# A new beginning for a fused linear-attention and two-layer kernel: fewer warm-up matmuls, moved state sums, loads behind the masks, and decay scans run backwards

## The reference, cut to what matters

```python
for t in range(S):                                   # attention, S = 768
    cur = einsum('bhd,bhe->bhde', u[None] * kt, vt)
    y[:, :, t] = einsum('bhd,bhde->bhe', rt, state + cur)
    state = wt[:, :, :, None] * state + einsum('bhd,bhe->bhde', kt, vt)
...
h = x @ w_in                                         # 384 -> 2048
g = h * clip(h + 3.0, 0.0, 6.0) / 6.0
x = g @ w_out                                        # 2048 -> 384
...
xn = x / sqrt(mean(x * x) + 1e-06) * rms_g
g = xn @ w_gate; val = xn @ w_val                    # 384 -> 1536, twice
out = (silu(g) * val) @ w_out2                       # 1536 -> 384
```

## Time and profile before

| | |
|---|---|
| median of 3 runs | 933.13 us (932.55 to 935.83) |
| the profiled execution | 935.66 us, of which 933.9 us are its span |
| PE busy | 921.6 us, 99% of the span |
| DVE, ScalarE (ACT), POOL busy | 521.3, 361.7, 291.9 us |
| moved by DMA | 60.40 MB |
| mean granted TensorE clock | 0.998 |

### The profile page before, as it was taken

How to read it: one execution, slowest core, us unless ns; L and a number is a source line. 1 busy time by engine, 2 the same in 40 slices (tenths; PEclk the granted TensorE clock), 3 DMA queues, 4 the chain that set the end, 5 groups by cost and what they waited for, 6 DMA issues and landing times.

```text
span 933.9 us, 17547 instructions
## 1 busy us (share of the span) xinstructions
PE 921.6 (99%) x7064; PEld 772.9 (83%) x7064; DVE 521.3 (56%) x752; ACT 361.7 (39%) x786; POOL 291.9 (31%) x244
## 2 busy tenths in 40 slices
PE   7999999999999999999999999999999999999998
PEld 7899988888888888888888888888888888888886
DVE  6888976566666666315774553553463373363332
ACT  4557454354444445336463123223223223223212
POOL 4789544454454444324351011011011001101000
PEclk9999999999999999999999999999999999999999
DMA  9874442233223231014221010010000001000000
GB/s 255 237 208 129 109 131 60 63 105 86 75 61 107 69 83 51 22 39 135 86 83 45 0 35 34 1 34 34 0 34 35 1 19 50 0 1 34 1 1 34
DMA packets 33008, 60.40 MB, mean 65 GB/s; under 512 B 6112, under 2 KB 19936, under 8 KB 32928
## 3 DMA queue, kind: packets, MB, share of 16 engines
q1 hardware_dynamic: 27104, 50.82, 18.7%
q10 hardware_dynamic: 5824, 8.47, 3.1%
HBM read 47.66 MB, written 9.44 MB: 61 GB/s over the span
## 4 chain that ended last, share of the span: by engine, by line
PE 93%; DVE 4%; issue 1%; DMA 1%; ACT 1%; SPq 1%; DVEq 0%; ACTq 0%
PE acc L1079 34%; PE bank L1050 11%; PE bank L1052 11%; PE bank L1051 11%; PE pair L1050 5%; PE pair L1051 5%; PE pair L1052 5%; DVE ki L731 1%; PE acc L1113 1%; PE pair L1132 1%; PE pair L1189 1%; PE pair L1161 1%; DVE cum L719 1%; PE bank L1068 1%; PE bank L1153 1%
## 5 line engine op out<-in xcount | busy, mean ns | idle before, releaser
L1079 PE MATMUL acc<-gs,w_dn 128*128 128x512 f32 (+1 forms) x1512 | 357.0, 382 | 1.2 <-issue 1.2
L1079 PEld LDWEIGHTS acc<-gs,w_dn 128*128 128x128 f32 x1512 | 272.9, 188 | 55.1 <-issue 1.3
L945 POOL TENSOR_TENSOR gs<-act_g,gs 128x512 fp32r<-128x512 f32 (+1 forms) x96 | 122.1, 1272 | 208.3 <-ACT gs L550 208.2
L1050 PE MATMUL bank<-xs,w_up 128*128 128x512 f32 (+1 forms) x459 | 171.9, 374 | 1.4 <-DVE state L762 1.2
L1052 PE MATMUL bank<-xs,w_up 128*128 128x512 f32 (+1 forms) x459 | 169.1, 368 | 0.0
L1051 PE MATMUL bank<-xs,w_up 128*128 128x512 f32 (+1 forms) x459 | 169.0, 368 | 0.0
L801 DVE SCALAR_TENSOR_TENSOR act_g<-act_u,bank 128x512 f32<-128x512 f32 (+1 forms) x112 | 67.5, 603 | 139.8 <-ACT act_u L542 139.8
L869 DVE TENSOR_TENSOR act_u<-act_u,bank 128x512 f32<-128x512 f32 x72 | 49.5, 688 | 146.8 <-ACT act_u L612 146.8
L542 ACT ACTIVATE act_u<-bank,half 128x512 f32<-128x512 f32 (+1 forms) x112 | 70.0, 625 | 150.8 <-PE bank L1052 139.9
L616 ACT ACTIVATE gs<-act_g 128x512 fp32r<-128x512 f32 x72 | 45.5, 632 | 155.9 <-DVE act_g L875 155.9
L1050 PEld LDWEIGHTS bank<-xs,w_up 128*128 128x128 f32 x459 | 86.4, 188 | 18.0 <-DVE state L762 1.6
(11 more groups left out here) (121 smaller groups left out, 1121.6 us busy)
## 6 DMA issues: line engine op xcount, KB each, us to landing
rkn<-in_rkN SPq DMA_DIRECT2D x22, 384.0 KB, 4.1
rkt<-in_rkT SPq DMA_DIRECT2D x44, 192.0 KB, 3.6
val<-in_valN SPq DMA_DIRECT2D x22, 256.0 KB, 3.0
x<-x_dram SPq DMA_DIRECT2D x6, 768.0 KB, 4.2
dec<-in_decT SPq DMA_DIRECT2D x46, 97.5 KB, 2.3
x_dram<-xo SPq DMA_DIRECT2D x5, 768.0 KB, 4.1
out<-xo SPq DMA_DIRECT2D x5, 768.0 KB, 3.3
raw_dn<-in_w_out SPq DMA_DIRECT2D x14, 192.0 KB, 4.8
```

Of the source, the lines that this page charges most:

```text
L945: pool.tensor_tensor(gs[:, f % GRING, 1, tok], act_g[:, f % 2, tok], gs[:, f % GRING, 0, tok].bitcast(F32), ALU.subtract).then_inc(s_glo, 1)
L1050: pe.matmul(dst, w_hi, x_hi, start=first, stop=False)
L1079: last = pe.matmul(ps_o[m][:, tok], w[:, wp, m * P:(m + 1) * P], gs[:, f % GRING, xp, tok], start=f == 0 and a == 0, stop=f == nf - 1 and ...
```

## The change

The decays of a chunk are no longer inverted. `prep_suffix` runs one scan backwards over the raw decays, and its result, the product of all decays behind a step, multiplies the keys directly. Its value at the chunk's start is the product over the whole chunk. `prep_prefix` takes the reciprocal of that one value (112 x 8 elements) and runs a second scan, forwards and in place over `dec`, that starts from it. POOL multiplies the queries by that. Per group, four reciprocals of 112 x 128 leave, and one scan of 112 x 520 and one reciprocal of 112 x 8 come. Because `dec` is overwritten, all groups load 64 rows of its first half (48 before), and its next load waits for `s_rd` instead of `s_cum` and stands one group later. `update_state` adds for every group, and `scale_state` runs for groups 0 and 1 too.

At the beginning PE issues 10 matmuls on ones (3 of 512 columns, 7 of 128) instead of 30 of 128. `sums(0)` and the DVE work behind it move into slice 0 of pass 0, and `keys(1)` into slice 2. The copies of values (`place_val3`), the first copy of keys and half of the second bonus fill move from ScalarE to DVE. ScalarE issues the loads of up slices 0 to 2 and of `u_b`. SP waits for both masks (`s_mask` 2) before it issues the loads of group 2, of up slice 3, and all behind them.

```diff
 # SyncE, before pass 0
-            landed(sp, ldR, 1, 2)
-            for b in range(PB):
-                sp.dma_start(u_b[...], ...)
-            load_rkn(2)
-            load_dec(2)
+            load_dec(2)
+            sp.wait_ge(s_mask, 2)
+            load_rkn(2)
+            load_up(sp, EARLY_UP)          # EARLY_UP = 3
+            load_dn(sp, 0)
             load_rk(2)
-            sp.wait_ge(s_ki, 2)
-            for f in range(FIRST_UP, FIRST_UP + 2):
+            load_dn(sp, 1)
+            for f in range(EARLY_UP + 1, FIRST_UP + 2):
                 load_up(sp, f)
                 load_dn(sp, f - 2)
             load_dec(3); load_rkn(3); load_rk(3)
 # VectorE
+            def prep_suffix(g):
+                dve.tensor_tensor_scan(suffix[...][:, ::-1], dec[::-1], first1[::-1], 1.0, ALU.mult, ALU.add)
+            def prep_prefix(g):
+                dve.reciprocal(whole1[0:DP, :, :, 0:1], whole(g))
+                dve.wait_ge(s_inv, g + 1)
+                dve.tensor_tensor_scan(dec, dec, whole1, 1.0, ALU.mult, ALU.add)
...
             for g in range(2):
-                prep_scan(g)
-                for part in range(2):
-                    prep_inv(g, part)
+                prep_suffix(g)
+                prep_prefix(g)
                 prep_k(g)
             dve.wait_ge(const, NCONST)
             for g in range(2):
-                mask_scores(g)
+                place_val3(g)
+            copy_first_keys()
+            mask_scores(0)
+            fill_half()
+            mask_scores(1)
...
                 if phase == INV1 and g + 3 < GROUPS:
-                    prep_scan(g + 3)
-                if phase in (INV1, INV2) and g + 3 < GROUPS:
-                    prep_inv(g + 3, phase - INV1)
+                    prep_suffix(g + 3)
+                if phase == INV2 and g + 3 < GROUPS:
+                    prep_prefix(g + 3)
 # GpSimd
-            pool.wait_ge(s_cum, 2)
             rk_mul(1)
 # TensorE
-            busy(20)
+            busy(3, 4)
+            busy(5, 1)
             bonuses(0)
-            busy(3)
             scores(0)
             keys(0)
-            busy(3)
+            busy(2, 1)
             bonuses(1)
-            sums(0)
-            busy(4)
             scores(1)
             outputs(0)
             outputs(1)
-            keys(1)
...
+                    if (e, f) == (0, 0):
+                        pe.wait_ge(s_bonus, PLACED)
+                        sums(0)
                     if (e, f) == (0, 2):
-                        sums_read(pe, 0)
+                        keys(1)
```

More of the change, by code:

```diff
@@ L99, in build @@
         first1 = sa("first1", [P, PAIRS, PB, T1])
[L100 removed]
+        whole1 = sa("whole1", [P, PAIRS, PB, T1])
+        suffix = sa("suffix", [P, 2, CHUNKS + 2])
         rd = sa("rd", [P, 2, PAIRS, PB, T])
@@ L160, in key_bank @@
         def key_bank(g):
-            return ps_h[g] if g < 2 else ps_c
+            return ps_h[0] if g == 0 else ps_c
         def sum_bank(g, b):
@@ L212, in columns, with after, whole @@
             return slice(g % B * C, (g % B + 1) * C)
-        def is_first(g):
-            return g < SETS
+        def after(g):
+            return suffix[0:DP, slot(g), 2:2 + CHUNKS].rearrange("p (c t) -> p c t", t=T1)[:, :, 0:T]
+        def whole(g):
+            return suffix[0:DP, slot(g), 0:CHUNKS].rearrange("p (c t) -> p c t", t=T1)[:, :, 1:2]
         def has_state(g):
@@ L658, in _ @@
                     act.activation(to[rows, :], of[rows, T * b:T * (b + 1)], ACT.Copy).then_inc(const, 1)
-            for f in range(FIRST_UP):
+            for f in range(EARLY_UP):
                 load_up(act, f)
-                if f < 2:
-                    load_dn(act, f)
+            for b in range(PB):
+                act.dma_start(u_b[T * b:T * (b + 1), :], u[b].partition_broadcast(T)).then_inc(ldU, 16)
             act.sem_inc(stX, 16)
@@ L665, in _ @@
             act.wait_ge(const, NCONST)
-            for g in range(2):
-                copy_bonus(g)
-                for part in range(2):
-                    fill_bonus(g, part)
-                place_val3(g)
-                if g == 0:
-                    copy_keys(0)
-            for g in range(2):
-                keep_last(g)
-            for f in range(2):
-                split_up(f)
+            copy_bonus(0)
+            for part in range(2):
+                fill_bonus(0, part)
+            copy_bonus(1)
+            fill_bonus(1, 0)
+            split_up(0)
             x1_hi(0, 0)
-            split_up(2)
+            split_up(1)
             x1_hi(1, 0)
-            copy_keys(1)
-            for f in range(3, FIRST_UP):
+            for f in range(2, FIRST_UP):
                 split_up(f)
@@ L846, in attention @@
                 if phase == PREP:
-                    if has_state(g) and not is_first(g):
+                    if has_state(g):
                         scale_state(g)
```

124 lines of the change are left out of this document (64 added, 60 removed).

## The result

The changed kernel takes **940.23 us** (median of 5, 939.9 to 943.45), the kernel before beside it 933.46 us (5 runs, 932.55 to 935.83): ratio 1.0073, 95% interval 1.0056 to 1.009. It is slower by 6.8 us. The forecast was 931.9 us, with 937.5 as its upper end.

The account below looks back on a forecast made before the run. The prediction took PE as the bound, under way for 921.6 of 933.9 us. Its terms, +1.1 (loads) - 2.0 (pass 1) - 0.3 (code) = -1.2 us, took 933.13 to 931.9 us, range 926.8 to 937.5.

Parts of the forecast that it names:

- the loads behind the masks: Beginning: loads held until the second mask bring up 6 late, at 32.1 us; +1.1 us at `up(0, 5)`, ends -1.5 and +4.0.
- second rival: Before `hidden(0, 3)`: PE starves after the loads restart and its clock falls; 938.8 us, chance 0.12.
- the scans: Decay preparation: a scan replaces costlier reciprocals on DVE; -2.0 us booked in pass 1, none booked at the beginning.
- DVE's chain: Beginning: the next limit if loads came faster; lighter DVE and the vanished hole give at most -3.5 us.
- Pass 1: Near 92 to 112 us: lighter DVE shortens PE's waits for the state; -2.0 us, ends -2.0 and 0.
- -0.3 for code: Later work: the 1.25 us code wait at 89.39 us goes, another may come; -0.3 us, ends -1.25 and +1.5.
- third rival: Pass 1: scans and POOL block each other at the shared port, the 2.0 us aren't gained; 935.2 us, chance 0.15.
- the hole: Ahead of slice 0: PE's 2.75 us wait for code in `outputs(0)` goes, slice 0 some 3 us earlier.
- the masks' end: DVE's beginning: the second mask ends at 18.1 us, ends 16.3 and 19.6, against 17.70 before.
- the load term: The step on loads held behind the masks: +1.1 us at `up(0, 5)`, upper end +4.0.
- fourth term: The prediction's words for the term lost if fewer PE instructions change nothing about code fetches.
- first rival: Beginning: loads are no limit, up 6 is in time; -3.5 - 2.0 - 0.8 = -6.3, 926.8 us, chance 0.24.

Follow-up runs that it names:

- e3: The kernel before with suffix and prefix scans in place of scan and reciprocals, old beginning and load order kept: 938.03 us, ratio 1.0054.
- e13: The changed kernel without the mask wait, with the wide full warm-up filling and scale_state(0) behind prep_k(2): 937.10 us, ratio 1.0049.
- e8: e1 with scale_state(0) moved behind sum_bonus(2) and prep_k(2): 937.13 us, ratio 1.0035.
- e1: The changed kernel without SP's wait for the masks, nothing else different: 938.18 us, ratio 1.0049.
- e17: e13 with POOL's r product of group 2 two weight splits later in POOL's order: 935.12 us, ratio 1.0014.
- e4: The changed kernel with the old inversion of the decays, one scan and four reciprocals: 940.48 us, ratio 1.0083.
- e11: The kernel before with its 30 warm-up matmuls cut to the changed kernel's 10: 932.31 us, ratio 0.9981.
- e16: The kernel before with e5's early hold of the loads and e11's thin warm-up filling: 931.54 us, ratio 0.9982.
- e6: e5 with the 30 warm-up matmuls made into 8 wide ones, nearly as many columns: 933.10 us, ratio 0.9989.
- e18: e13 with group 0's state sums and the state update back ahead of slice 0: 938.67 us, ratio 1.0051.
- e7: e1 with as many warm-up columns as the kernel before, in 8 wide matmuls: 937.84 us, ratio 1.0039.
- e5: The kernel before with group 2's loads and all behind them held until POOL's second query product: 933.01 us, ratio 0.9988.
- e2: The kernel before with the wait for both masks put ahead of group 2's natural-order key loads: 935.33 us, ratio 1.0029.

## Why the prediction was wrong, point by point

**Two steps of the sum failed. The first is "the loads behind the masks".** Its mechanism was right and its size wrong: +1.1 us was forecast at `up(0, 5)` and +4.0 measured, the very upper end. The mask ended at 18.09 us (18.1 forecast), the DMA engines stood still, and the restart ran at 218 and then 289 GB/s. But up 6 was there at 33.9, not 32.1. From 18.1 to 33.9 us 4.2 x 218 + 11.6 x 289 = 4.3 MB had moved, all but one packet of it on SP's queue. That is a mean of 271 GB/s, and 273 was forecast: the rate was right. But only 3.38 MB stood up to up 6's end in SP's order, so some 0.9 MB that were issued behind it moved ahead of its last byte. The forecast had counted none of that. So 1.8 us; 0.3 more from the split to the end of `hidden(0, 3)` (2.7 against 2.4); and 0.7 from there to slice 5 (3.0 against 2.3), where six matmuls of `down_raw` took 2.93 us at a clock that had just fallen. That was the second rival ("the restart starves PE so long that the clock falls", 0.12). Its point of decision, up 6 after 34 us, was missed by 0.1 us (33.9), yet what it describes happened, and its 938.8 us is the nearest of the forecast's times.

**The second is the scans, and by the runs it is the larger.** The sum had them as a gain (-2.0 in pass 1) and at nothing in slices 0 to 5; alone they cost 0.54%, 5 us (e3), of which the trace has 3.65 by `up(0, 5)`. So without the wait `up(0, 5)` is still at 36.3 to 38.4 (e13, e8, e1). The forecast had looked at up 6 alone and called DVE's chain "next", at -3.5, as if DVE ran beside POOL there. The other limit, POOL's r product ahead of the splits and the row of splits that holds DVE, was not in the sum; e17 sizes its place in POOL's order at 1.75 us in the trace and 0.35% (some 3 us) by the ratios. Late loads and scans hide behind each other: all of the change but the scans loses 7.7 us (e4), the scans alone 5.0, and both together 6.8. So no removal of one gives its full size. What e17 still loses (0.14%) was not followed.

**Pass 1: -2.0 forecast, and -0.3 for code.** Both are one stretch, from `up(0, 5)` to `up(2, 0)`: -2.3 forecast, -0.4 measured. It is +0.55 to `up(0, 8)` (the clock), +1.0 to `up(1, 0)` (the scan of 5.20 us) and -1.9 from there. The size of the last was right, but its cause is not the lighter DVE alone: e3 gets 1.9 us there with the scans and all instructions, and e11 gets 1.9 us with all reciprocals and 80 instructions fewer. The waits of the earlier trace rows hang on each other, and two reasons to remove one of them were booked as two gains. The third rival ("the shared port", 0.15) named the place and gave -2.0 not gained; it looked for PE's wait at `g_lo`, which took 0.3 us, and it was at the state, 2.1 us.

**Right:** the hole goes (no "issue" wait of over 0.3 us in `outputs`), the DMA share near 0 ahead of the second mask, ScalarE's waits for raw_up with the longest ahead of `split_up(6)`, a backward scan at 1.24 us alone and 2.21 beside POOL, and nothing behind `up(2, 0)` but 0.7 us, nearly all at the end. Slice 0, at 20.5, came half a microsecond behind the forecast's 19.5 to 20. That the masks' end was met is luck, of two errors that cancel: the keys of group 1 were done at 14.16 and not 15.1, and the work from there to the second mask took 3.9 us and not 3.0 (two value copies 1.30 instead of 0.5). DVE ahead of pass 0, after:

```profile
4.88 1.24 DVE L714 TENSOR_TENSOR_SCAN suffix<-dec,first 112x520 f32<-112x520 f32 x1 [2.74 <-DMA dec<-in_decT]
...
9.20 2.21 DVE L714 TENSOR_TENSOR_SCAN suffix<-dec,first 112x520 f32<-112x520 f32 x1
...
13.50 0.66 DVE L735 TENSOR_TENSOR ki<-rkt,suffix 112x512 f32<-112x512 f32 x1
14.08 1.30 DVE L767 TENSOR_SCALAR val<-val 128x96 f32<-128x96 f32 x2
...
17.36 0.73 DVE L742 COPY_PREDICATED att<-mask,acc 128x512 f32<-128x512 int32 x1
```

**The base.** The sum was put on a median of 933.13 by way of one profiled execution that lay 2.5 us above it, and it was assumed that the changed kernel's would lie as far above its own. It lay 0.3 below. That is 2.9 of the 8.3 us between forecast and result; the terms are the other 5.5 (2.9 at `up(0, 5)`, 1.9 to `up(2, 0)`, 0.7 behind it). A range whose upper end took the load term's +4.0 and left pass 1 at 0 would have been 933.1 + 4.0 = 937.1, and not held it either. (The prediction names the -0.3 for code a "fourth term"; its sum has three. The -0.8 for code in its first rival is worked out nowhere.)

The Trainium skill (SBUF — State Buffer, SBUF: two separate sides) has a DVE instruction with two SBUF inputs and a GpSimd instruction exclude each other for a whole instruction. The traces agree (0.68 against 3.11 us) and add that the wait does not end with one instruction: the scan of 5.20 us ended only behind the fourth of POOL's operations in a row.

## What to carry to other kernels

A hold on a queue of loads is priced by how long the queue stands still, by all that stands between it and the last byte a later stage waits for, and by what is issued behind that byte and moves with it: released 3.3 us later, the same hold went from free (0.9988) to some 3 us (1.0029). Before work is moved or made cheaper on one engine, look at the engine that shares its port: an operation that waits there, with short ones queued behind it, turns into a row that holds its neighbour. And where two edits each remove the same wait, book it once; test each alone before adding them up.

## What the runs showed of the hardware that I had not expected

- A two-input operation of DVE can wait through several of POOL's in a row: 5.20 us for a scan of 1.24, 3.11 for a product of 0.68, 3.60 for a scan under splits. A one-input reciprocal of the same length never did: 1168 to 1171 ns in 20 instances.
- A granted clock of 0.50 for 6.8 us of PE's beginning (e11, e16), and in e1 for 17.1, cost nothing that the ratios show. The traces show 0.4 to 1.6 us of it at `up(0, 5)` where no wait for code takes it up.
- PE's first wait for code stands at a count and not at a place in the program. In nine traces an "issue" wait of 0.3 to 2.75 us ends at PE's 450th or 451st instruction: in `outputs(0)` in the kernel before, in `outputs(1)` in e6, e11 and e18, in `sums(0)` in e7 (1.96 us). In all nine PE goes on 1.4 to 1.5 us after the end of a code packet, so the wait depends on when that packet comes: at 17.54 us in the kernel before (2.75 us of wait), at 15.17 in e5 (0.30), where the loads are held. In e2 and e16, held as well, it came at 14.93 and 15.20 us and there was no wait. The load on the queues isn't all of it: with the same hold as e5 and e16, it came at 18.09 in e6 (2.12 us of wait), and why was not followed.
- Eighty instructions fewer also shifted the later waits: the 1.25 us "issue" wait of the earlier trace rows is gone in e11, and pass 1's stretch took 47.2 us and not 49.1. The Trainium skill (Runtime: NRT & Kernel Launch, Instruction fetch mechanics) gives PE's side room for 2048 instructions; the hole of the earlier trace rows came behind the 441st that had started by 17.8 us, so in this case that room did not spare PE the wait.
